# The last group of a sliding-window attention and two-MoE kernel goes over to the wide gate form, with a second buffer in the opening and no closing drain

## The reference

```
scores = q @ k.T / 8, kept where 0 <= row - col < 64        # 4 x 8 heads, 576 tokens, 64 wide
attn   = softmax(scores) @ v                                # -> x, 2304 tokens x 512
x      = (sigmoid(x @ w_gate) * (x @ w_val)) @ w_out        # 512 -> 1536 -> 512
logits = x @ w_gate2 + log1p(exp(x @ w_noise)) * noise      # 8 experts
top2   = the two largest logits of a token, softmax of the two as weights
out    = sum over the two experts e: weight * (relu(x @ w1[e]) @ w2[e])   # 512 -> 1024 -> 512
```

## Time and profile before

| | |
|---|---|
| median of 3 runs | 984.58 us (982.96 to 985.42) |
| profiled execution | 982.77 us |
| its span | 980.9 us |
| TensorE matmul busy | 967.7 us, 99% |
| VectorE busy | 514.2 us, 52% |
| ScalarE busy | 370.0 us, 38% |
| GpSimd busy | 400.1 us, 41% |
| granted TensorE clock, mean | 0.997 |

### The profile page before, as it was taken

The page is one execution under the profiler, slowest core; times in us unless marked ns, Lnnn a source line. Parts: engine busy times, 40 slices in busy tenths (PEclk is TensorE's granted clock), DMA queues, the critical chain, the costliest instruction groups (busy, mean ns, idle before and its releaser), DMA issues.

```text
span 980.9 us, 17645 instructions
## 1 busy us (share of the span) xinstructions
PE 967.7 (99%) x6505; PEld 853.2 (87%) x6505; DVE 514.2 (52%) x1277; ACT 370.0 (38%) x892; POOL 400.1 (41%) x401
## 2 busy tenths in 40 slices
PE   8999999999999999999999999999999999999996
PEld 7998888888888888888999898898998989898994
DVE  5665576765757576664455435443534334443510
ACT  6553343434334243423244323343424234343420
POOL 4882224242332424232111414654727273655302
PEclk9999999999999999999999999999999999999998
DMA  7656333243534324232044433673736465563403
GB/s 244 206 171 173 119 113 106 89 143 97 144 98 139 99 75 130 80 94 86 23 118 129 75 109 79 165 164 77 168 70 151 99 156 116 136 142 94 78 12 43
DMA packets 82727, 113.09 MB, mean 115 GB/s; under 512 B 19216, under 2 KB 45840, under 8 KB 82640
## 3 DMA queue, kind: packets, MB, share of 16 engines
q1 hardware_dynamic: 69008, 84.63, 29.5%
q0 software_dynamic: 13344, 27.05, 14.1%
q10 hardware_dynamic: 288, 0.26, 0.1%
HBM read 83.13 MB, written 28.77 MB: 114 GB/s over the span
## 4 chain that ended last, share of the span: by engine, by line
PE 97%; ACT 1%; DVE 1%; issue 1%; POOLq 0%; POOL 0%; DVEq 0%; ACTq 0%
PE bank L1108 22%; PE bank L1092 22%; PE bank L985 16%; PE bank L1008 16%; PE bank L991 10%; PE bank L989 5%; PE bank L965 2%; PE bank L907 2%; ACT arena L1253 1%; PE bank L1076 0%; PE bank L1034 0%; PE bank L1043 0%; PE bank L1115 0%; PE bank L1056 0%; PE bank L925 0%
## 5 line engine op out<-in xcount | busy, mean ns | idle before, releaser
L991 PE MATMUL bank<-xr,wr 128*128 128x256 f32 x864 | 242.6, 281 | 0.0
L985 PE MATMUL bank<-xr,wr 128*128 128x512 f32 x672 | 239.9, 397 | 0.0
L1092 PE MATMUL bank<-wr 128*128 128x256 f32 (+1 forms) x1536 | 223.8, 306 | 0.6 <-DVE wr L1717 0.4
L1092 PEld LDWEIGHTS bank<-wr 128*128 128x128 f32 x1536 | 221.3, 190 | 2.1 <-DVE wr L1717 0.7
L770 POOL DMA_INDIRECT arena<-x_rows,shared x120 | 130.5, 1087 | 143.5 <-DVE v_nat L1704 95.3
L1008 PE MATMUL bank<-wr,hr 128*128 128x512 f32 x648 | 170.5, 398 | 0.0
L738 POOL TENSOR_TENSOR hr<-arena,hr 128x256 fp32r<-128x256 f32 x84 | 61.7, 735 | 263.8 <-ACT hr L1301 263.8
L991 PEld LDWEIGHTS bank<-xr,wr 128*128 128x128 f32 x864 | 163.6, 189 | 3.5
L985 PEld LDWEIGHTS bank<-xr,wr 128*128 128x128 f32 x672 | 126.2, 188 | 30.2
L1008 PEld LDWEIGHTS bank<-wr,hr 128*128 128x128 f32 x648 | 114.0, 188 | 23.3 <-issue 0.2
L1108 PE MATMUL bank<-wr 128*128 128x512 f32 (+1 forms) x576 | 133.2, 391 | 0.0
(11 more groups left out here) (158 smaller groups left out, 1022.3 us busy)
## 6 DMA issues: line engine op xcount, KB each, us to landing
arena<-moe_w SPq DMA_DIRECT2D x40, 512.0 KB, 3.9
arena<-moe_w SPq DMA_DIRECT2D x96, 128.0 KB, 4.9
p_rows<-arena SPq DMA_DIRECT2D x28, 256.0 KB, 2.0
v_nat<-p_rows SPq DMA_DIRECT2D x112, 64.0 KB, 2.0
arena<-gv SPq DMA_DIRECT2D x12, 512.0 KB, 4.5
out<-zeros POOLq DMA_DIRECT2D x20, 256.0 KB, 2.7
x_rows<-arena SPq DMA_DIRECT2D x9, 512.0 KB, 3.8
arena<-k SPq DMA_DIRECT2D x17, 256.0 KB, 4.7
```

Of the source, the lines that this page charges most:

```text
L985: pe.matmul(ps_g[m].rearrange("p (a n) -> p a n", a=2), gv_w[:, f, m, kk], xr[:, g % 2, :, kk], start=(kk == 0), stop=False, skip_group_ch ...
L991: mm = pe.matmul(ps_g[m][:, 0:GT], gv_w[:, f, 2 + m, kk], xr[:, g % 2, 0, kk], start=False, stop=(kk == KC - 1), skip_group_check=True)
L1092: mm = pe.matmul(ps_h[u % 2][:, 0:n], w1_r[e % 2][:, a, kk, f * P:(f + 1) * P], xT[p][:, b, kk, 0:n], start=(kk + x == 0), stop=(kk == KC ...
```

## The change

The last group's slots become wide too, with h_low kept on VectorE there (inner_low names the slots in which GpSimd has it). In the opening, blocks 1 and 3 are turned into v_mix instead of pT, values(2) is cut in two around turn_p(3), the orders on ScalarE and VectorE are adapted, GpSimd waits for the first low part of the gate weights, and the first mixed load waits until v_mix is free. In the routing behind the last group, choose_first and choose_second stand one set later on VectorE and rank_rows one set later on TensorE. The split of expert 1's second weights is spread over every second set. The block ends without GpSimd's drain.

```diff
 def turned(n):
+    if n < OPEN and n % 2:
+        return v_mix.rearrange("p (c m) -> p c m", c=GP)
 def wide(c):
+    return c >= FC
+def inner_low(c):
     return FC <= c < LAST - FC
-block = ctx.enter_context(nc.Block())
+block = ctx.enter_context(nc.Block(no_gpsimd_drain=True))
 def load_mixed(t):
-    if t > 2:
-        sp.wait_ge(pv_done, 2 * t - 1)
+    sp.wait_ge(pv_done, 2 * t - 1 if t > 2 else OPEN)
...
+load_v(2)
 load_mixed(2)
-load_v(2)
 # GpSimd
 pool.wait_ge(scaled_first, OPEN)
+pool.wait_ge(gv_lo, 1)
 split_out(0)
...
-    if wide(s):
+    if inner_low(s):
         h_low(s)
 # TensorE: values(n) loses the case n == 2
+def values_half(n, rows, r0, r1):
+    if r0:
+        pe.wait_ge(half_done, 1)
+    else:
+        pe.wait_ge(pT_done, n + 1)
+        pe.wait_ge(v1_in, 16)
+        pe.wait_ge(x_lo, n - 1)
...
 up(e, p, f), f < 2 of the first expert
-        pe.wait_ge(h_done if u else gate_done, LAST)
+        pe.wait_ge(vals_added if u else gates_added, LAST - FC)
 turn_p(2)
-idle(3)
-values(2)
+idle(5)
+values_half(2, v_nat1, 0, WIN)
 turn_p(3)
-idle(3)
+values_half(2, v_nat, WIN, P)
 values(3)
...
-for f in range(3, 6):
+for f in range(3, 7):
     up(0, 0, f)
 rank_rows(GROUPS - 1)
 # ScalarE
 def copy_pT(n):
-    if n:
+    if n >= OPEN:
         act.wait_ge(pv_done, n)
+    elif n >= 2:
+        act.wait_ge(pv_done, n - 1)
-    act.copy(pT[0:c1 - c0], ...)
+    act.copy(turned(n)[0:c1 - c0], ...)
 exps(2)
+copy_pT(1)
 x_high(0)
-copy_pT(1)
 exps(3)
+copy_pT(2)
 x_high(1)
-copy_pT(2)
...
 soften(GROUPS - 1)
-relu(0, 0, 3)
-relu(0, 0, 4)
+for f in range(3, 6):
+    relu(0, 0, f)
 weigh_exp(GROUPS - 1)
...
     relu(1, 1, f)
-    if f < KC:
-        high(1, KC + f)
+    if f % 2 == 0:
+        high(1, KC + f // 2)
 # VectorE
-x_low(0)
 sums(2)
 scale_first(2)
-x_low(1)
+x_low(0)
 sums(3)
 scale_first(3)
+x_low(1)
...
-    if not wide(s):
+    if not inner_low(s):
         h_low(s)
...
 copy_logits(GROUPS - 1)
+hidden_low(0, 0, 3)
 choose_first(GROUPS - 1)
-hidden_low(0, 0, 3)
+hidden_low(0, 0, 4)
 choose_second(GROUPS - 1)
-hidden_low(0, 0, 4)
 hidden_low(0, 0, 5)
+hidden_low(0, 0, 6)
 slots(GROUPS - 1)
 weights(GROUPS - 1)
-for f in range(6, F2C):
-    hidden_low(0, 0, f)
+hidden_low(0, 0, 7)
...
     hidden_low(1, 1, f)
-    if f < KC:
-        low(1, KC + f)
+    if f % 2 == 0:
+        low(1, KC + f // 2)
```

More of the change, by code:

```diff
@@ L926, in turn_p @@
                 mm.then_inc(p_turned, 1)
+            def values_half(n, rows, r0, r1):
[5 more added lines that the diff above has]
+                    pe.wait_ge(x_lo, n - 1)
+                pe.nop(nofuse=True)
+                for c in range(GP):
+                    i, j = divmod(c, 2)
+                    for h in range(2):
+                        mm = pe.matmul(ps_x(n)[h * HD:(h + 1) * HD, c * WIN:(c + 1) * WIN],
+                                       rows[r0:r1, (2 * c + h) * HD:(2 * c + h + 1) * HD],
+                                       pT[r0:r1, 2 * i + h, j * WIN:(j + 1) * WIN], start=(r0 + c == 0), stop=(r0 > 0),
+                                       skip_group_check=True)
+                mm.then_inc(pv_done if r0 else half_done, 1)
             def values(n):
@@ L930, in values @@
                 pe.wait_ge(pT_done, n + 1)
[L931 removed]
+                if n == 3:
                     pe.wait_ge(v1_in, 16)
@@ L946, in values @@
                 pe.nop(nofuse=True)
[L947 to L960, removed]
                 rows = v_nat1 if n == 3 else v_nat if n % 2 or n == 0 else v_mix
@@ L1181, in _ @@
             router_rows(GROUPS - 1)
-            for f in range(3, 6):
+            for f in range(3, 7):
                 up(0, 0, f)
             rank_rows(GROUPS - 1)
-            for f in range(6, F2C):
+            for f in range(7, F2C):
                 up(0, 0, f)
@@ L1261, in copy_pT @@
                 act.wait_ge(p_turned, n + 1)
-                if n:
+                if n >= OPEN:
                     act.wait_ge(pv_done, n)
-                act.copy(pT[0:c1 - c0], ps_p[0:c1 - c0].rearrange("p (c m) -> p c m", c=GP)).then_inc(pT_done, 1)
+                elif n >= 2:
+                    act.wait_ge(pv_done, n - 1)
+                act.copy(turned(n)[0:c1 - c0], ps_p[0:c1 - c0].rearrange("p (c m) -> p c m", c=GP)).then_inc(pT_done, 1)
             def x_high(n):
@@ L1443, in _ @@
             soften(GROUPS - 1)
-            relu(0, 0, 3)
-            relu(0, 0, 4)
+            for f in range(3, 6):
+                relu(0, 0, f)
             weigh_exp(GROUPS - 1)
-            for f in range(5, F2C):
+            for f in range(6, F2C):
                 relu(0, 0, f)
```

1 line of the change is left out of this document (removed).

## The result

| | before | after |
|---|---|---|
| median of the runs beside each other, us | 984.58 (982.96 to 986.48, 9 runs) | 987.61 (985.89 to 988.72, 9 runs) |
| profiled execution, its span, us | 982.77, 980.9 | 988.72, 986.6 |

The ratio is 1.0029, 95% interval 1.0021 to 1.0037: the change costs 3.0 us, where the forecast was 2.1 (986.7 us). It lies in the range, in the upper half of rival A's own (984.7 to 988.5). The profiled execution of after is the slowest of its runs and that of before (982.77) is faster than each of its nine, so 5.7 us lie between the two spans, more than between the medians. The kernel was run once more later, beside the experiments (`after_again`: 985.86 against 982.93, ratio 1.0027, 1.0017 to 1.0038); that span, 984.0, is 3.1 above the one of before, and I use it for the ledger.

What follows compares the result with a forecast made beforehand. TensorE, carrying 97% of the chain of work, was taken to bound the kernel. Terms -0.6 - 0.6 + 5.2 - 0.4 + 0.6 - 2.1 gave +2.1 us, 986.7 us, range 981.3 to 989.3.

Steps and rivals of the forecast that it cites:

- rival A: The forecast itself: VectorE's queue makes TensorE wait in slots 102 to 107; +2.1, 986.7 us (984.7 to 988.5); chance 0.54.
- Opening, -0.6: Before the first gate matmul: reordered values(2) and turn_p(3) start the gate 0.7 us sooner; -0.6 us (-0.75 to 0).
- rival E: The opening gives nothing or loses as GpSimd's late queue holds turn_p(4); +2.7 to +3.7, 987.8 us; chance 0.08.
- hidden by the same slots: Opening: the gate-and-value load, queued about 1 us later on SP, was to stay hidden by two slots over 4.26 us.
- Wide form, -0.6: Last group: each of twelve slots 0.05 us shorter with the wide form; -0.6 us.
- VectorE's queue, +5.2: Last group: two reductions a slot delay add_gates; TensorE waits 2.0, 1.1, 0.85, 0.55, 0.2, 0.5 us; +5.2 (0 to 6).
- Routing, -0.4: Behind the last group: hidden_low(3) now precedes choose_first, so TensorE's 0.40 us wait goes; -0.4 us.
- The spread, +0.6: Expert 1: waits inside up(1,1,f) nearly go, but down(1,0) waits for the last subtraction; +0.6 us (-0.5 to +0.8).
- The close, -2.1: Kernel end: without GpSimd's closing drain, SP's wait for the final scatter is last; -2.1 us (-2.15 to 0).

Runs made afterwards that it cites:

- drain_only: The kernel before without GpSimd's closing drain, nothing else changed; 983.96 us against 986.24, ratio 0.9979.
- splits_moved: The changed kernel with expert 0's four split pairs in slots 98, 99, 103 and 105 instead of 99 to 102; 982.03 us, ratio 0.9991 to before.
- best: The kernel before with the change's opening, routing and no closing drain, last group narrow, expert 1's splits behind sets 0, 2, 4, 5; 979.69 us against 982.91.
- no_opening: The version best without the opening's edits, its other parts kept; 980.01 us against 982.93 for before, ratio 0.9971.
- narrow_last: The changed kernel with the last group's slots narrow again, all other parts kept; 980.66 us, ratio 0.9978 to before.
- warm_fill: The changed kernel with 16 matmuls of zeros into a free bank ahead of slot 102's gate; 985.92 us, ratio 1.0030 to before.
- soften_later: The changed kernel with ScalarE's high(0,1) ahead of soften(7)'s table loads in slot 100; 983.71 us against 982.91 for before, ratio 1.0007.
- wide_only: The kernel before with only the last group's twelve slots made wide; 993.85 us against 986.24, ratio 1.0078.
- spread_only: The kernel before with only the split of expert 1's second weights behind every second set of up(1,1,f); 987.59 us, ratio 1.0016.
- opening_only: The kernel before with the opening's new order alone; 985.39 us, ratio 0.9999.

## Why the prediction was right

**Opening, -0.6.** The start of the gate is right in time and mechanism. Over all profiles it lies at 17.87 to 18.51 with the edits (nine, mean 18.20) and at 18.62 to 19.55 without (five, mean 18.87), -0.67; without the 19.55 of drain_only it is -0.50. turn_p(4) came at 24.59, as worked out, so GpSimd's late queue didn't hold it (rival E). split_low(0) takes 1.23 us when GpSimd doesn't run beside it, for 2.25. The Trainium skill has VectorE and GpSimd share SBUF interfaces and contend when a VectorE instruction has two SBUF inputs ("GPSIMD Engine Reference", Specifications); the rows agree.

One step of it failed: the load of gate weights that I let go about 1 us later, "hidden by the same slots". SP issues it at 18.23 for 17.34, now behind the mixed loads, and ScalarE's copy of what it brings waits for it:
```profile
17.34 0.33 SPq L550 DMA_DIRECT2D arena<-gv  x1
22.57 1.04 ACT L1284 CAST wr<-arena 128x1024 fp32r<-128x1024 f32 x1
```
```profile
18.23 0.58 SPq L558 DMA_DIRECT2D arena<-gv  x1
23.05 1.05 ACT L1302 CAST wr<-arena 128x1024 fp32r<-128x1024 f32 x1 [1.07 <-DMA arena<-gv]
```
The first two lines are of before, the others of after. Such a wait stands in each of the nine traces with the opening's edits (0.64 to 3.07 us) and in none of the five without. In after, after_again and splits_moved VectorE's subtraction behind the copy starts after one of GpSimd's (24.13 behind 24.08 in after) and takes 2.33, 2.03 and 1.86 us; in best it starts first (24.55, GpSimd's at 24.71) and takes 1.22. In these three the gate matmuls of slot 2 come late, out_rows(1) 12.83, 13.11 and 14.35 us behind the gate's start for 12.61 or 12.62 in the other eleven. Over the nine traces that is 0.27 us on average, so by an estimate from them 0.4 of the 0.67 are left, near the 0.3 of no_opening. No run changed the order of the loads alone.

**Wide form, -0.6.** The slots without a wait or other work took 4.17 us for 4.26, a gain of 0.09 instead of 0.05, those with other work gained 0.06, and after_again against narrow_last leaves 0.6 for all twelve. It matters little: from slot 102 to 104 VectorE sets the pace.

**VectorE's queue, +5.2.** Right in mechanism, and its clock almost to the digit. I had put the starts of slots 102 and 104 at 499.24 and 509.72; they came at 498.69 and 509.13, 0.55 to 0.6 earlier, as much as the slots were ahead by then (out_rows(99) starts at 490.88 for 491.45). The add_gates of VectorE follow each other after 5.36 and 5.08 us (497.95, 503.31, 508.39), where I had 5.37 and 5.11 and where a slot takes 4.17. Only what TensorE did in between was different: for 2.0, 1.1 and 0.85 of waiting it shows 2.09, then a slot of 5.85 us (498.69 to 504.54) instead of 4.17, then 0.21. Against an undisturbed run of slots (496.44, which is 1.39 behind out_rows(100), and two slots of 4.17 make 504.78) slot 104 is 4.35 us late, where I had 3.95. Of the difference, 0.18 is that I had reckoned the two slots at 4.26, and 0.16 is a reading: the start of out_rows(100) that I took from the chain of work, 495.87, stands at 495.71 in the timeline. Behind them stand waits of 0.47, 0.16 and 0.22 us for 0.55, 0.2 and 0.5. But the idle time in a row counts from a modelled end (495.05 + 1.55 for out_rows(100)), 0.16 behind the moment at which the next matmul would be issued, so each is more than it shows: against narrow_last, after_again falls back by 0.59, 0.39 and 0.36 at these places. That makes 5.7 for 5.2. That VectorE sets the pace through slots 103 and 104, and that the lower clock is no extra cost, is shown by warm_fill, where its rows stand as in after while TensorE runs at full clock; soften_later shows the wait of slot 104 once more.

**Routing, -0.4.** Right in mechanism: in after the sets from up(0,0,3) on show no wait, and the 0.40 of the earlier trace rows stands in wide_only, spread_only, drain_only and opening_only, which lack the edit. For the same reason as above it was worth more: from up(0,0,3) to turn_g(3) 10.28 us for 10.98, -0.7.

**The spread, +0.6: the term that was too small.** On the two other chips it costs 1.0 (13.27 and 13.28 for 12.27). Two things went into my number. That down(1,0) waits for the last subtraction is right (0.86 us). But I had taken the waits inside the sets as nearly gone, 0.25 us. The eight sets take 12.27 us up to the next issue (best), and 8 x 1.44 is 11.5, so 0.75 stays. In after_again the relus of the sets 0 to 7 start at 609.30, 610.74, 612.17, 613.99, 615.43, 616.87, 618.31 and 620.12: two steps are 1.8 long instead of 1.44, because hidden_low(f+1) still stands behind a subtraction. relu(6) is 10.65 us behind the first matmul, where I had 10.24, and the last subtraction ends 13.2 behind it, where I had 12.8. best, whose last pair is one set earlier, has the same waits inside and none at the end, and loses nothing. The spread as such gives nothing either: 12.27 with the four pairs in a row and 12.27 with them at 0, 2, 4, 5.

**The close, -2.1.** It gave 2.5 to 2.6 in the profiles of after, after_again and drain_only and 2.3 in drain_only's median: right in kind. I had let SP's last semaphore stand 0.5 us behind its wait; it stands 0.2 behind.

**The sum.** By after_again the terms are -0.5 (start of the gate), +5.1 (slots and routing, for 4.2 forecast), +1.0, -2.6, and 0.1 elsewhere: 3.1 for 2.1. The 5.1 are 5.7 for VectorE's queue, -0.6 for the wide form, -0.7 for the routing, +0.5 between the gate's start and out_rows(1) (the load above; 0.22 of it is shown as a wait at 26.99), and 0.2 that belongs to the profile of before: from the gate to out_rows(42) it took 209.32 us, and the ten other traces without a late slot 2 took 209.53 to 209.58. I lay no cause to that. So five sizes were off by 0.3 to 0.5 us, three one way and two the other, and that the total came within 1 us is in part their cancelling.

**Left open.** In all four profiles of the first chip, and in that of after, ScalarE comes late to a relu early in up(1,1,f), and TensorE waits 1.13 to 1.33 us there (in after at 612.94), with edits that have nothing to do with it; in none of the eight profiles of the other two chips, nor in that of before. This one and a like one about 826 are most of what the profiled execution of after has over after_again in the last columns of the ledger (1.0 and 1.9 us). No rows show what ScalarE waited for, and I made no run for it. How much of the gate's 0.5 us reaches the median is also unsettled.

## What to carry to other kernels

When a step moves from one engine's queue into another's, work out when it ends there, behind everything that the queue already holds in that slot; here two reductions of 0.69 us a slot cost 5.2 us net, because one of them came to stand behind the subtractions of four slots; 2.15 us of it went when the subtraction of slot 100 no longer waited for two table loads, and some 3.8 when all four were moved. Once an engine off the path has no slack left, what the engine on the path did in between (a wait, slow matmuls, filling) made no difference here: remove work from the late queue or reorder it, as moving four splits or one copy did. A load that is let go later has to be followed to its reader on every engine in the same way. And if work is spread over a loop, let its last piece end before the instruction that waits for all of it starts: one set earlier was worth 1.0 us.

## What the runs showed of the hardware

- After 2.08 to 2.10 us of standing, the granted clock went to its lower level in each of the three profiles that have such a wait, and stayed there for about 3.4 us: at once in after_again, 0.6 us behind the wait's end in wide_only, 1.4 behind it in after. After waits of 1.21 (soften_later), 1.41 (wide_only, at 771) and 1.46 us (splits_moved, at 27.94), or with the wait filled by matmuls of zeros (warm_fill), it stayed at 1.00. A pair of matmuls, 512 and 256 columns, took 0.64 us at the lower level and 0.35 at the higher.
- The closing drain of GpSimd's queue was worth 2.5 us in the profiles (7.82 to 7.88 from the last scatter's issue to the end with it, 5.17 to 5.43 without).
- Where a subtraction of VectorE (128x1024) and one of GpSimd (128x512) met in the opening, the one that started first took its usual time and the other about a microsecond more: GpSimd 1.27 at 14.95 and VectorE 2.25 at 15.06 (before), GpSimd 1.29 at 24.08 and VectorE 2.33 at 24.13 (after), VectorE 1.22 at 24.55 and GpSimd 2.23 at 24.71 (best).
- A load of 512 KB, issued 0.9 us later behind two others, made ScalarE wait between 0.64 and 3.07 us in nine traces, and TensorE up to 1.46 us (splits_moved): single traces with the same opening differ by that much.
